# One core's attention and expert program: another order of the input loads, and the TensorE's loop over heads turned by one step

## The reference

```python
scores = scale * np.matmul(q, k.transpose(0, 1, 3, 2))
scores = scores + bias.transpose(2, 0, 1)[None, :, :, :]
scores = scores - np.max(scores, axis=-1, keepdims=True)
attn = np.exp(scores)
attn = attn / (np.sum(attn, axis=-1, keepdims=True) + 1e-09)
return np.matmul(attn, v).astype(np.float32)
...
for e in range(E):                      # mixture of experts, 2304 tokens of 512
    mask = e_idx == e
    h = np.maximum(x[mask] @ w1[e], 0.0)
    out[mask] = gate_w[mask, None] * (h @ w2[e])
...
h = np.maximum(np.maximum(x @ w1, x @ w2), x @ w3)
return (h @ w_out).astype(np.float32)
```

## Time and profile before

| quantity | value |
|---|---|
| median of 3 runs (lowest to highest) | 966.75 us (965.48 to 970.1) |
| the profiled execution's own time | 966.75 us |
| span of its trace | 965.0 us |
| bias table, attention, the rest | to 66 us, 66 to 311 us, from 311 us |
| busy in the whole span: PE, DVE, ACT, POOL | 92%, 56%, 35%, 37% |

### The profile page before, as it was taken

How to read it: one execution, slowest core, us unless ns; L and a number is a source line. 1 busy time by engine, 2 the same in 40 slices (tenths; PEclk the granted TensorE clock), 3 DMA queues, 4 the chain that set the end, 5 groups by cost and what they waited for, 6 DMA issues and landing times.

```text
span 965.0 us, 24953 instructions
## 1 busy us (share of the span) xinstructions
PE 888.1 (92%) x9749; PEld 765.0 (79%) x9749; DVE 540.8 (56%) x1004; ACT 341.4 (35%) x750; POOL 353.9 (37%) x346
## 2 busy tenths in 40 slices
PE   6967889999997379999999999999999999999998
PEld 3536767788786258888888888889999999999997
DVE  7966889999995845444444574444514233333231
ACT  6964667777875414230000340242210111101100
POOL 0948555343332378670000781586420202010100
PEclk9987999999999579999999999999999999999999
DMA  4769678777765787551000462465110102000001
GB/s 143 270 210 249 158 227 207 214 195 206 181 158 147 252 269 206 170 167 63 23 22 22 152 208 78 129 185 167 33 66 1 66 1 66 1 33 2 33 1 33
DMA packets 71466, 120.98 MB, mean 125 GB/s; under 512 B 26632, under 2 KB 30872, under 8 KB 69352
## 3 DMA queue, kind: packets, MB, share of 16 engines
q1 hardware_dynamic: 48360, 74.20, 26.6%
q10 hardware_dynamic: 17616, 30.27, 10.5%
q0 software_dynamic: 5424, 15.58, 5.0%
HBM read 93.12 MB, written 26.90 MB: 124 GB/s over the span
## 4 chain that ended last, share of the span: by engine, by line
PE 62%; POOL 2%; DVE 2%; issue 1%; ACT 0%; ACTq 0%
PE moe_banks L1525 23%; PE moe_banks L1446 13%; PE moe_banks L1480 13%; PE moe_banks L1542 8%; PE moe_banks L1464 2%; POOL slots L1261 2%; PE moe_banks L1431 1%; PE moe_banks L1508 1%; DVE slots L1676 0%; POOL x_tok L1295 0%; DVE in_lane L1614 0%; ACT x_tok L1373 0%; PE moe_banks L1413 0%; ACT slots L1351 0%; DVE xT L1651 0%
## 5 line engine op out<-in xcount | busy, mean ns | idle before, releaser
L1261 POOL TENSOR_TENSOR slots<-x_tok,slots 128x512 fp32r<-128x512 f32 (+1 forms) x116 | 140.9, 1248 | 155.1 <-ACT slots L1351 154.9
L1525 PE MATMUL moe_banks<-yT,slots 128*128 128x384 f32 x1080 | 193.1, 334 | 0.0
L1525 PEld LDWEIGHTS moe_banks<-yT,slots 128*128 128x128 f32 x1080 | 188.0, 188 | 0.5
L1351 ACT CAST slots<-x_tok 128x512 fp32r<-128x512 f32 (+1 forms) x116 | 67.9, 602 | 255.5 <-PE moe_banks L1446 128.4
L1446 PE MATMUL moe_banks<-slots,xT 128*128 x600 | 146.5, 401 | 1.2 <-issue 0.6
L1480 PE MATMUL moe_banks<-slots,hT 128*128 x600 | 140.3, 389 | 0.7 <-POOL slots L1261 0.7
L1446 PEld LDWEIGHTS moe_banks<-slots,xT 128*128 128x128 f32 x600 | 113.2, 192 | 25.3 <-issue 1.9
L1480 PEld LDWEIGHTS moe_banks<-slots,hT 128*128 128x128 f32 x600 | 112.6, 188 | 24.3 <-issue 1.0
L806 ACT ACTIVATE probs<-probs,negmax 128x576 f32<-128x576 f32 x144 | 110.9, 771 | 44.2 <-DVE negmax L756 43.1
L756 DVE CUSTOM_DVE_ANT_0 probs<-s_ps,bias 128x576 f32<-128x576 f32 x144 | 104.6, 753 | 33.9 <-PE s_ps L636 13.9
L675 PE MATMUL o_ps<-pT,v_raw 32*64 32x160 f32 (+1 forms) x4608 | 99.9, 300 | 7.4 <-issue 5.2
(11 more groups left out here) (171 smaller groups left out, 1068.7 us busy)
## 6 DMA issues: line engine op xcount, KB each, us to landing
x_tok<-in_moe_w ACTq DMA_DIRECT2D x96, 256.0 KB
v_raw<-in_v SPq DMA_DIRECT2D x64, 288.0 KB, 5.4
bias_table<-staged SPq DMA_DIRECT2D x36, 296.0 KB, 2.9
bias<-bias_table SPq DMA_DIRECT2D x32, 288.0 KB, 5.9
result_rows<-y SPq DMA_DIRECT2D x25, 256.0 KB, 2.0
q_raw<-in_q SPq DMA_DIRECT2D x16, 320.0 KB, 3.6
k_raw<-in_k SPq DMA_DIRECT2D x16, 288.0 KB, 3.0
x_rows_by_tile<-x_tok SPq DMA_DIRECT2D x16, 288.0 KB, 5.2
```

The source lines that it names most:

```text
L1261: nc.gpsimd.tensor_tensor(rest, raw(n, rows), near.bitcast(F32), ALU.subtract).then_inc(part_done(e, part)[0], 1)
L1351: nc.scalar.copy(near, raw(n, rows)).then_inc(near_done, 1)
L1525: last = nc.tensor.matmul(u_ps[m], final_weight(far, slots, m, d, a, f), yT[:, c, d, :], start=(d == 0 and k == 0), stop=(d == KD - 1 and ...
```

## The change

It has two parts.

1. **SP's order.** In heads 1 to 6 both units' keys and queries are now issued before both units' values; the store of the results of unit 1 of two heads earlier stands right behind the bias rows (ahead of the queries and keys; in the last head ahead of both values). Before, the values of unit 0 stood between the two pairs of keys and queries, and the store between them and the values of unit 1. Number and size of the transfers are the same.
2. **PE's loop.** PE now uses `heads_loop` as DVE and ACT do: head 0 written out, a loop of heads 1 to 6, head 7 written out. The body forms in step s the scores of the step after it. The order of the matmuls is the same as before; what moves is where the loop turns (before: between `outputs` and the first scores of the next head; now: after the last three blocks of values that follow those scores) and that the last head is no longer a pass of the loop. The waits for `turn_gate_in` and `gate_placed` stand a few instructions later.

```diff
-            def values_rows(it, u):
-                sp.wait_ge(o_filled, unit(it - 1, u) + 1)
-                load_values(sp, it, u)
+            def values_rows(it):
+                for u in range(2):
+
+                    sp.wait_ge(o_filled, unit(it - 1, u) + 1)
+                    load_values(sp, it, u)
...
                 bias_rows(it)
-                keys_queries(sp, it + 1, 0)
-                values_rows(it, 0)
-                keys_queries(sp, it + 1, 1)
                 if it == 2:
                     store_rows(sp, 0, 1)
-                values_rows(it, 1)
+                for u in range(2):
+                    keys_queries(sp, it + 1, u)
+                values_rows(it)
                 store_rows(sp, it - 1, 0)
             with sp.Fori(3, HEADS - 1) as it:
                 bias_rows(it)
-                keys_queries(sp, it + 1, 0)
-                values_rows(it, 0)
-                keys_queries(sp, it + 1, 1)
                 store_rows(sp, it - 2, 1)
-                values_rows(it, 1)
+                for u in range(2):
+                    keys_queries(sp, it + 1, u)
+                values_rows(it)
                 store_rows(sp, it - 1, 0)
             bias_rows(HEADS - 1)
-            values_rows(HEADS - 1, 0)
             store_rows(sp, HEADS - 3, 1)
-            values_rows(HEADS - 1, 1)
+            values_rows(HEADS - 1)
             store_rows(sp, HEADS - 2, 0)
...
-            def head(it, first):
+            def head(it, first, last):
                 for u in range(2):
                     previous = (it, 0) if u else (it - 1, 1)
-                    if not (first and u == 0):
-                        scores(it, u, 0)
-                    if not first:
-                        values(it - 1, u, VALUES[COMB])
-                    for s in range(COMB):
-                        scores(it, u, s + 1)
+                    for s in range(STEPS):
+                        if not (last and u == 1 and s == COMB):
+                            scores(*after(it, u, s))
                         if s == COMB - 1 and not first:
                             outputs(it - 1, u, FULL * unit(it, u) + FULL)
-                        if s in VALUES and not (first and u == 0):
+                        if not (first and u == 0) and s in VALUES:
                             values(*previous, VALUES[s])
+                if first:
+                    pe.wait_ge(turn_gate_in, 16)
+                    pe.wait_ge(gate_placed, 1)
...
-            head(0, True)
-            pe.wait_ge(turn_gate_in, 16)
-            pe.wait_ge(gate_placed, 1)
-            with pe.Fori(1, HEADS) as it:
-                head(it, False)
-            values(HEADS - 1, 0, VALUES[COMB])
+            heads_loop(pe, head)
             values(HEADS - 1, 1, VALUES[0])
```

## The result

The changed kernel takes 1004.55 us in the median of four runs (1001.99 to 1008.23), the kernel before 966.34 us in the runs beside it. The ratio is 1.039, with a 95% interval of 1.034 to 1.044. I had forecast 990 us and a range of 978 to 999. The direction was right and so were the mechanisms (late values, a slow clock behind the stall, instruction loads in the written-out head); three of the sizes were not, and the measured time lies outside the range. The profiled execution took 999.16 us with a span of 997.4 us, less than any of the four; against the profile of before it is 32.4 us longer.

The account below looks back on a forecast made before the run. The prediction took PE and DVE, in step without reserve, to bound the attention. Late values 21.9, the loop's turn 0 and the written-out head 1.5 made 23.4 us on 966.75: 990 us, range 978 to 999.

Parts of the forecast that it names:

- What bounds the attention: Attention: PE and DVE both nearly always busy, at most 0.9 us reserve a unit; no known cover behind it.
- Part 1 as a mechanism: SP's queue: unit 0's values wait behind the second queries and keys, making PE stall; 21.9 us in all.
- The stall: PE at unit 0's values, head 3: wanted at 176.11, landed at 179.4, so 3.3 us (2.7 to 3.7).
- head 2: Attention, third head: values landed at 150.4, wanted at 147.40, a stall of 3.0 us; cost 3.4 us.
- upper bound of 3.7 us: PE's wait for unit 0's values: top of the 2.7 to 3.7 us given around 3.3 us.
- queued behind: SP's queue: unit 1's values go out at 175.2 behind unit 0's late quartet and land near 185.
- The clock: PE behind the 3.3 us stall: clock drops, 80 values and 12 scores take 4.2 us instead of 2.8.
- Head 1: Attention, second head: values landed 116.6 to 117.3, wanted at 116.48, a stall of 0.1 to 0.8; cost 0.5 us.
- Part 2, the turn: PE's loop, turning 6 times at its new place: bounded by 0.5 us either way each, taken as 0.
- Part 2, the written-out head: PE's last head, outside the loop: idle times for instruction loads, 1.5 us (0 to 5).
- more than the sum: Rival: longer stalls behind the next unit's quartet, or instruction loads stalling the last head; 998 to 1003 us, chance 0.07.
- heads 3 to 6: Attention: DVE late by 4.5 us in each of these four, 18.0 us (12.4 without the drop of clock).

Follow-up runs that it names:

- split2: Kernel before, but in heads 1 to 6 the last two of unit 0's four value loads stand behind the second k and q: 967.23 us, ratio 1.007.
- hold1: Kernel before with SP's changed order, unit 1's values held until POOL has the next keys done: 993.79 us, ratio 1.025.
- pe_only: Kernel before with only PE's loop changed, SP's order as before: 975.57 us, ratio 1.008.
- unroll_only: Kernel before with the last head written out behind PE's loop, loop body and turn as before: 976.75 us, ratio 1.011.
- unroll_two: Kernel before with heads 6 and 7 written out behind PE's loop, loop body and turn as before: 980.83 us, ratio 1.013.
- split3: Kernel before, but in heads 1 to 6 the last of unit 0's four value loads stands behind the second k and q: 963.69 us, ratio 0.999.
- split1: Kernel before, but in heads 1 to 6 three of unit 0's four value loads stand behind the second k and q: 979.56 us, ratio 1.021.
- busy_wait: Kernel before with SP's changed order and 16 unused matmuls ahead of PE's wait for unit 0's values: 987.11 us, ratio 1.019.

## Why the prediction was wrong, step by step

- **What bounds the attention**: right. PE and DVE in step, no reserve, and a head pays its stall less 0.15 us (`split2`). The sum behind the attention did not cover any of it.
- **Part 1 as a mechanism**: right. SP's order alone costs 28 us; six waits for `v_raw`, none before; the store costs nothing.
- **The stall**: mis-sized, 3.3 us (3.0 in head 2) against 3.7 to 5.1. I took the landing of a quartet behind k and q, 8.1 us from the first issue. The quartet here stands closer behind them and landed later than in any of the three cases I had; q itself landed after 3.5 us instead of 3.1. It measured 8.5 in heads 4 and 5 and more in the others. The upper bound of 3.7 us has no row either: the latest landing that I worked out, 179.5, gives 3.4. In head 3 the next quartet, close behind, made it longer still (`hold1`); that neighbour I had ruled out as "queued behind".
- **The clock**: that it would drop was right, in every head; its price was mis-sized. I took 1.4 us a head, from a row in which 80 records took 2.52 us. They took 2.98, the scores 1.80, and the next values were slow in part: 5.4 us at 0.55, 2.0 to 2.3 us a head. The trace of before had a dearer row too, behind the idle time of 1.84 us:

```profile
107.11 2.74 PE L675 MATMUL o_ps<-pT,v_raw 32*64 32x160 f32 x80
```

- Together a head of 3 to 6 pays 5.9 to 7.0 us instead of 4.5, 25.4 instead of 18.0; head 2 pays 5.4 instead of 3.4.
- **Head 1**: the 0.5 us look right beside 0.7, but for a wrong reason. The stall there is 4.1 us, not 0.1 to 0.8. In the kernel before, PE idled 1.84 us just ahead of q's issue and ran slowly behind it, which put the use of the values later and left q's issue where it was; I read the gap between these two as if it were fixed. From the head's first values to the issue of q are 8.4 us before and 8.1 now, but to the use 17.6 and 13.7. That idle time is gone when the values are late. In the four kernels with the old place of the values it is 1.8 to 2.2 us (before, `pe_only`, `unroll_only`, `unroll_two`), in `split3` 0.99, and in the seven kernels with two or more late loads it does not occur. The instruction load at that place is held up by the loads of values ahead of it: counted from the head's first values, it shows on q8 at 4.8 to 5.5 us in those four kernels, at 3.5 in `split3`, at 2.5 in `split2`, and at 1.8 to 2.0 in the six with three or four late loads. So the 0.7 us are a stall and a slow clock less this gain: luck.
- **Part 2, the turn**: right, it costs nothing that shows (`unroll_only` against `pe_only`).
- **Part 2, the written-out head**: the step that failed most, about 7 of the 14.8 us by which the forecast fell short; part 1 missed by about 6. I had 0 to 5 us and took 1.5; it measured 8 to 10 us in the medians (8.6 in `pe_only`, 9.8 in `unroll_only`). The idle times are what the first passes had shown, two of about 2 us. I left out that they bring the slow clock, though the rows for that stood in the same list, and halved them for a lighter traffic that did not make them shorter. The Trainium skill's page "Runtime: NRT & Kernel Launch", section "Instruction fetch mechanics", holds the cost of fetching in sequence to be mostly hidden, and by that this head would have cost about nothing. The runs go against it in this kernel: seven loads on q8 from the start of that head on where the kernel before has three, idle times of 2.02 and 2.13 us, and 8.9 us in the profiled execution.
- **The range**: it ended 5.6 us below the median. The case "more than the sum" had 998 to 1003 us and a chance of 0.07, and its own working does not fit: 5 us on top of 990 are 995. The terms of heads 3 to 6, of head 2 and of the written-out head were bounded one by one, but all three hold the price of the slow clock, and missed on the same side.

## What to carry to other kernels

An issue order on a queue is a set of deadlines: moving a load behind another's wait costs nothing until the landing of the last byte passes the moment of use. From there on, in a stage without reserve like this one, each microsecond counts once per pass of the loop. Work out that landing from the measured case that stands closest behind its neighbours in the queue, and take it as a lower bound when the new place is closer still. Let every term with idle time of PE carry a price of the slow clock too: where the runs priced it, it was 1.3 to 2.4 us a stall, and it came behind every stall of 2.71 us or more and behind some shorter ones. In this kernel a loop whose code stays loaded was worth keeping whole: each head written out cost 6 to 9 us.

## What I had not expected of the hardware

- **The slow clock does not follow from the length of the rest alone.** 2.60 us of rest left the clock full and 2.71 did not (`split1`); 1.84 us brought it down in the kernel before, and 1.83 us did not in `split2`. Even 1.48 us did in head 1 of `split2`, while the 1.48 us of `busy_wait` above left it full:

```profile
111.73 2.84 PE L677 MATMUL o_ps<-pT,v_raw 32*64 32x160 f32 x80 [1.48 <-DMA v_raw<-in_v]
```

Once down, it stayed so for 3.7 us (before, at 106.3) to 6.5 us (`pe_only`, 299.2 to 305.7 at 0.52). What decides between a rest that brings it down and one that does not stays open.
- **Idle times in code that runs for the first time.** 1.1 to 2.7 us each in the written-out heads, two to three in a head of some 28 us, and none while the loop turns. PE went on 2.5 to 3.5 us behind the instruction load ahead of each. In head 1 the load and with it the idle time also answer to what stands ahead in the DMA queues (1.8 to 2.2 us behind a quartet of values, 0.99 behind three loads, none behind two or fewer).
- **One load of 128 partitions from four times the same 32 rows** ran at 70 to 115 GB/s; with loads of 32 partitions on their way the queues moved 225 GB/s (180.1 to 185.1 us in the changed kernel).
